# q and k of tiles 8 to 27 turned in 32 by 32 blocks by the vector engine instead of by the tensor engine

## What is computed

```python
for c in range(nc):                       # chunks of 32 tokens
    k_full = concat(mem_k, k[16 tokens before the chunk .. 8 behind it])
    v_full = concat(mem_v, v[the same tokens])
    scores = scale * q_c @ k_full^T
    a = exp(scores - max); a = a / (sum(a) + 1e-9)
    out[chunk] = a @ v_full
x = out, as (3072 tokens, 512)
h = x @ w_in;  solu = h * softmax(h);  ln = (solu - mean) / sqrt(var + 1e-6) * g_ln
x2 = ln @ w_out
h2 = x2 @ w2_in;  g = h2 * clip(h2 + 3, 0, 6) / 6;  result = g @ w2_out
```

## Time and profile before

| | us |
|---|---|
| median of 3 runs | 903.2 |
| lowest and highest | 901.8, 905.31 |
| the profiled execution, its own time | 903.9 |
| its span, from first to last instruction | 901.8 |
| PE busy in the span | 882.5 |
| DVE busy | 677.2 |
| ACT busy | 468.9 |
| POOL busy | 264.4 |

### The profile page before, as it was taken

The page is one execution under the profiler, slowest core; times in us unless marked ns, Lnnn a source line. Parts: engine busy times, 40 slices in busy tenths (PEclk is TensorE's granted clock), DMA queues, the critical chain, the costliest instruction groups (busy, mean ns, idle before and its releaser), DMA issues.

```text
span 901.8 us, 16537 instructions
## 1 busy us (share of the span) xinstructions
PE 882.5 (98%) x6146; PEld 796.7 (88%) x6146; DVE 677.2 (75%) x1100; ACT 468.9 (52%) x1112; POOL 264.4 (29%) x327
## 2 busy tenths in 40 slices
PE   7999999999999999999999999999999999999998
PEld 6788989888988989899888888888799999999998
DVE  5898878888777878757685545555898887979784
ACT  5777565656565654537574555545754333333331
POOL 4473554563341454550122324223610000000000
PEclk9999999999999999999999999999999999999999
DMA  9895265555454464577733333333996435354341
GB/s 211 184 214 127 63 181 164 181 164 179 136 141 131 140 224 133 161 258 275 272 115 133 128 124 129 131 140 115 352 363 238 153 99 159 97 160 142 116 141 47
DMA packets 145017, 149.26 MB, mean 166 GB/s; under 512 B 92725, under 2 KB 104501, under 8 KB 143925
## 3 DMA queue, kind: packets, MB, share of 16 engines
q1 hardware_dynamic: 132205, 103.06, 38.4%
q0 software_dynamic: 7920, 38.94, 12.3%
q10 hardware_dynamic: 4824, 6.34, 2.1%
HBM read 90.77 MB, written 57.54 MB: 164 GB/s over the span
## 4 chain that ended last, share of the span: by engine, by line
PE 85%; DVE 9%; DMA 2%; ACT 2%; issue 1%; SPq 0%; DVEq 0%; ACTq 0%
PE banks L1405 25%; PE banks L1144 24%; PE banks L1096 23%; PE banks L1041 3%; PE banks L1111 3%; DVE prob L1801 2%; PE banks L1049 2%; PE banks L1070 2%; PE banks L993 2%; PE banks L1087 2%; DVE score L1771 1%; DVE small L1779 1%; DMA xs_raw<-x_scratch 1%; DMA gs_raw<-g_scratch 1%; DVE y_t L1762 1%
## 5 line engine op out<-in xcount | busy, mean ns | idle before, releaser
L1405 PE MATMUL banks<-vs,gs 128*128 128x256 f32 x2016 | 242.6, 283 | 1.7 <-DMA vs<-v_split_scratch 1.4
L1405 PEld LDWEIGHTS banks<-vs,gs 128*128 128x128 f32 x2016 | 242.2, 192 | 2.1 <-DVE gs L1762 1.6
L1144 PE MATMUL banks<-xs,ws 128*128 128x512 f32 x1008 | 230.8, 390 | 0.8 <-ACT part L1541 0.8
L1144 PEld LDWEIGHTS banks<-xs,ws 128*128 128x128 f32 x1008 | 188.1, 188 | 42.4 <-issue 2.7
L1719 ACT CAST gs<-gs_raw 128x1792 fp32r<-128x1792 f32 x48 | 81.4, 1696 | 124.3 <-DVE gs_raw L2115 124.3
L1096 PE MATMUL banks<-y_t,w_out 128*128 128x384 f32 x768 | 140.8, 338 | 0.0
L1096 PEld LDWEIGHTS banks<-y_t,w_out 128*128 128x128 f32 x768 | 132.7, 188 | 0.9
L1096 PE MATMUL banks<-w_in,x_t 128*128 128x512 f32 x480 | 114.7, 394 | 0.2 <-DVE solu L1848 0.2
L1488 ACT ACTIVATE prob<-score,small 96x128 f32<-96x128 f32 x256 | 99.3, 392 | 19.1 <-DVE small L1779 17.8
L2115 DVE TENSOR_TENSOR gs_raw<-gs_raw 128x256 f32<-128x256 f32 x192 | 82.1, 428 | 32.3 <-DMA gs_raw<-g_scratch 27.5
L1096 PEld LDWEIGHTS banks<-w_in,x_t 128*128 128x128 f32 x480 | 88.6, 188 | 19.0 <-DVE solu L1848 0.4
(11 more groups left out here) (105 smaller groups left out, 1039.6 us busy)
## 6 DMA issues: line engine op xcount, KB each, us to landing
g_scratch<-part SPq DMA_DIRECT2D x96, 256.0 KB, 2.0
gs_raw<-g_scratch SPq DMA_DIRECT2D x45, 512.0 KB, 4.0
x_scratch<-x_out ACTq DMA_DIRECT2D x32, 192.0 KB, 2.1
v_in<-in_v_dram SPq DMA_DIRECT2D x24, 240.0 KB
out_dram<-o_stage SPq DMA_DIRECT2D x11, 512.0 KB, 5.6
q_in<-in_q_dram SPq DMA_DIRECT2D x28, 192.0 KB, 3.0
v_split_scratch<-v_split POOLq DMA_DIRECT2D x3, 1792.0 KB, 7.7
ws<-w_split_scratch SPq DMA_DIRECT2D x21, 256.0 KB, 5.5
```

Of the source, the lines that this page charges most:

```text
L1144: mm = pe.matmul(ps, ws[:, W_OF[i], a, kc, :], xs[g][X_OF[i]][:, m, kc, :], start=(fresh and x == 0), stop=(x == len(passes) - 1), skip_gr ...
L1405: mm = pe.matmul(m_ps[i][:, s, :], gs[x][:, a, G_OF[i], s * P:(s + 1) * P], vs[p][:, m, V_OF[i], :], start=(p == 0 and s == 0 and y == 0), ...
```

## The change

q and k of tiles 8 to 27 are no longer loaded with tokens on the partitions. A tile of q is loaded by 12 DMAs, one for each of its three chunks of 32 tokens and each of four partition groups (`split_rows`). Group e takes, for every second head, 32 of the 64 features of 32 tokens: 32 partitions (tokens) x 4 head pairs x 32 features, in runs of 128 bytes, 16 KB a DMA. So every 32 by 32 block lies in the partition group in which its transposed values belong. DVE then transposes the blocks in place of their partition group, one instruction for q and one for k (`turn_blocks`), straight into `q_t` and `k_t`. k takes 12 DMAs too, and 24 where a batch begins (tiles 8, 16 and 24), since there the memory rows, the 16 and the 8 rows beside come in DMAs of their own. The DMAs of these 20 tiles are 240 for q and 276 for k; before it was 20 for q and, with 17 joined tiles of which two need a second one, and three whole windows of three, 28 for k.

PE's eight transposes of each of the 20 tiles go, and with them ACT's copies from PSUM. ACT keeps the copy of the 24 old columns (`join_k`). PE's probabilities no longer wait for ACT's copies out of the two banks. The scores of tile n now wait for DVE's blocks of tile n (`blocks_turned`) and for the joined columns.

```diff
+        def by_blocks(n):
+            return TILES <= n < NA - AHEAD
...
+            def split_rows(dst, c, r, src, b, lo, rows, here):
+                for e in range(NQUAD):
+                    sp.dma_start(dst[CHUNK * e + r:CHUNK * e + r + rows, :, c, :],
+                                 src[b, e // 2::2, lo:lo + rows, CHUNK * (e % 2):CHUNK * (e % 2 + 1)]
+                                 .rearrange("h r d -> r h d")).then_inc(here, 16)
...
+                if by_blocks(n):
+                    for c in range(TQ // CHUNK):
+                        split_rows(q_split[t % 2], c, 0, q, b, TQ * t + CHUNK * c, CHUNK, q_in_here[t % 2])
+                    return
...
-                pe.wait_ge(q_in_here[s], 16 * (TILES // 2 * b + t // 2 + 1))
-                turn(turn_ps[0], q_in[:, s], TQ)
-                pe.wait_ge(k_in_here[s], k_in_count(n))
-                if is_joined(n):
-                    turn(turn_ps[1], k_in[0:TQ, s], TQ)
-                else:
-                    turn(turn_ps[1], k_in[:, s], NK)
...
+                elif by_blocks(n):
+                    pe.wait_ge(blocks_turned, 2 * (n - TILES) + 2)
+                    pe.wait_ge(qk_copied, 2 * TILES + joined_before(n + 1))
+                    q_of, k_of = q_t, k_t[n % 2]
...
+            def turn_blocks(n):
+                if not by_blocks(n):
+                    return
+                s = n % 2
+                dve.wait_ge(q_in_here[s], q_in_count(n))
+                dve.wait_ge(scores_done, 2 * n)
+                nc.vector.transpose(q_t[:, :, :].rearrange("p h t -> p (h t)"),
+                                    q_split[s][:, :, :, :].rearrange("p h c d -> p (h c d)")).then_inc(blocks_turned, 1)
+                dve.wait_ge(k_in_here[s], k_in_count(n))
+                cols = slice(NK - TQ if is_joined(n) else 0, NK)
+                nc.vector.transpose(k_t[s][:, :, cols],
+                                    k_split[s][:, :, cols.start // CHUNK:, :].rearrange("p h c d -> p h (c d)")
+                                    ).then_inc(blocks_turned, 1)
...
                 moments_of(3)
+                turn_blocks(TILES)
...
                     if w["own"]:
                         norm_probs(n)
+                        turn_blocks(n + 1)
                     if w["mm1"]:
                         max_hidden(MPG * (i - 1) + u)
```

More of the change, by code:

```diff
@@ L121, in attention_solu_hardswish @@
         k_ahead = [at(f"k_ahead{e}", (198, 200, 202, 188)[e], [P, KD, NK], F32) for e in range(AHEAD)]
+        q_split = [at(f"q_split{s}", 136 + 2 * s, [P, KD, TQ // CHUNK, CHUNK], F32) for s in range(2)]
+        k_split = [at(f"k_split{s}", 140 + 2 * s, [P, KD, NK // CHUNK, CHUNK], F32) for s in range(2)]
         q_back = [at(f"q_back{s}", 136 + 2 * s, [P, KD, TQ], F32) for s in range(2)]
@@ L369, in raw_count, with joined_before, q_loads, q_in_count @@
             return 16 * sum(1 + LOADS[ahead_tile(x)] for x in range(e % 2, e + 1, 2))
+        def by_blocks(n):
+            return TILES <= n < NA - AHEAD
         def is_joined(n):
-            return n >= TILES and n % TILES > 0 and not is_ahead(n)
+            return by_blocks(n) and n % TILES > 0
+        def joined_before(n):
+            return sum(is_joined(x) for x in range(n))
+        def q_loads(n):
+            return 3 * NQUAD if by_blocks(n) else 1
+        def q_in_count(n):
+            return 16 * sum(q_loads(x) for x in range(n % 2, n + 1, 2))
         def k_loads(n):
-            if is_joined(n):
-                return 2 if n % TILES == TILES - 1 else 1
+            if by_blocks(n):
+                return NQUAD * (3 if is_joined(n) else 6)
             return 1 if is_ahead(n) else LOADS[n % TILES]
@@ L473, in load_k @@
                     return
[L474 to L480, removed]
+                if by_blocks(n):
+                    split, here = k_split[t % 2], k_in_here[t % 2]
+                    if t == 0:
+                        split_rows(split, 0, 0, mem_k, b, 0, NMEM, here)
+                        split_rows(split, 0, NMEM, k, b, 0, LEFT, here)
+                        split_rows(split, 0, NMEM + LEFT, k, b, 0, RIGHT, here)
+                    for c in range(TQ // CHUNK):
+                        lo = TQ * t + RIGHT + CHUNK * c
+                        split_rows(split, c + 1, 0, k, b, lo, min(CHUNK, S - lo), here)
                     return
@@ L1051, in turn_half, with turn_probs @@
                 mm.then_inc(prob_turned, 1)
-            def turn_probs(n, behind_qk):
+            def turn_probs(n, banks_read):
                 for half in range(2):
-                    if behind_qk and not is_ahead(n + 1):
-                        pe.wait_ge(qk_copied, 2 * n + 3 + half)
-                    elif not behind_qk and half == 0:
+                    if not banks_read and half == 0:
                         pe.wait_ge(y_lo_done, 2 * MPG * (NG - 1))
@@ L1308, in batch @@
                     if w["own"]:
-                        turn_qk(b if kk else b - 1, (kk - 1) % TILES, i, u)
+                        turns_read(b if kk else b - 1, (kk - 1) % TILES, i, u)
                     if w["mm2"]:
@@ L1662, in batch @@
                         high_x(n - 1, (kk - 2) % TPG, (kk - 2) // TPG % 2)
-                    if not last and not is_ahead(n + 1):
-                        copy_qk(n + 1)
+                    if is_joined(n + 1):
+                        join_k(n + 1)
                     if w["mm1"]:
```

44 lines of the change are left out of this document (21 added, 23 removed).

## The result

The changed kernel takes 954.4 us, the median of four runs (953.3 to 956.3); the kernel before took 903.2 us beside it. The ratio is 1.056, with a 95% interval from 1.053 to 1.059: 51 us slower, where 901.9 us was forecast, and 38 us outside the range. From here on a number such as "1.016 (1.011 to 1.021)" is the ratio to the kernel before on the same chip with its 95% interval, and "+2.3" means 2.3 us later than before.

What follows compares the result with a forecast made beforehand. PE, busy 882.5 of 901.8 us, was taken as the bound. Terms -2.3 + 6.2 - 2.0 - 2.4 + 1.8 gave 1.3 us gained, hence 901.9 us expected as median; range 896 to 916.

Steps and rivals of the forecast that it cites:

- tile 8: Start of tile 8's scores: blocks turned behind the first batch's moments, DVE without slack; a loss of 2.3 us.
- pair 10, 11: Hidden product's end to tile 11's scores, through DVE's moments and a scaling held up by POOL: a loss of 2.0 us.
- pair 14, 15: Scaling as long as tile 10's; maximum 0.7 us later, blocks cost 0.37: a loss of 1.1 us.
- pair 18, 19: Scaling as long as tile 10's; maximum 0.94 us later, blocks cost 0.37: a loss of 1.3 us.
- pairs 22, 23 and 26, 27: Tile pairs free of POOL: a gain of 0.9 us each, 1.8 together.
- The loads: SP's 516 DMAs at 0.36 us an issue, 210 us with v and stores, fit in 257 us: costed at nothing.
- SP becomes the engine that is waited for: Slower rival, SP's queue: at 0.50 us an issue 24 us late, 926 us; at 0.58, 967 us; chance 0.17.
- D: On DVE, how far a tile's two transposes push what stands behind them: 0.94 us, bounds 0.3 to 1.8.
- The clock: Rival: PE idles before tile 8's scores and tile 10's probabilities, clock halves: some 3 us, 905 us; inside the forecast's 0.50.
- covered tiles: Nine tiles where PE's projection hides DVE's turning: each keeps its 0.66 us, 6.2 us gained in all.
- Absorbed delays: Faster rival: pairs lose nothing and each tile but 8 brings 0.66 us; 10 us gained, 893 us; chance 0.16.

Runs made afterwards that it cites:

- two loads, behind scaling: Changed kernel with q and k of tiles 8 to 27 each loaded by one DMA (from w_in, wrong values), turning as changed: 918.3 us, 1.016.
- two loads, narrowed GpSimd: Changed kernel with two loads a tile, turning as changed, GpSimd's mixing and splitting narrowed to 8 columns for all but the first items: 905.2 us, 1.003.
- two loads, idle time: Changed kernel with two loads a tile, both turns moved into DVE's idle stretches: 903.3 us, 1.000.
- shapes run: Kernel before plus 24 unused DMAs a tile in tiles 8 to 27, their rows and runs varied from tile to tile: 958.5 us, single run.
- q alone in idle time: Kernel before with only q of tiles 8 to 27 loaded by blocks and turned by DVE, in DVE's idle time: 902.3 us, 0.998.
- 15 turns: Kernel before with only q of 15 of the 20 tiles loaded by blocks and turned by DVE in idle stretches: 901.6 us, 0.998.

## Why the prediction was wrong, point by point

One table carries most of it: by how much the start of each tile's scores is later than the start of those before it, less the same in the kernel before, in us, from the traces.

| scores of | forecast | two loads, behind scaling | two loads, narrowed GpSimd | two loads, idle time | changed kernel |
|---|---|---|---|---|---|
| tile 8 | +2.3 | +2.3 | +2.3 | +0.1 | +2.3 |
| 9, 12, 13, 16, 17, 20, 21, 24, 25 | -6.2 | +0.8 | -2.9 | -0.4 | +18.8 |
| pair 10, 11 | +2.0 | +1.5 | +1.8 | +0.2 | +5.7 |
| pair 14, 15 | +1.1 | +4.5 | +2.2 | +1.0 | +6.4 |
| pair 18, 19 | +1.3 | +4.2 | -1.7 | +0.9 | +4.4 |
| pairs 22, 23 and 26, 27 | -1.8 | -0.5 | -1.9 | -0.7 | +8.7 |

**The loads: the step that failed.** The prediction wrote: "I take 0.36, since each new DMA stands behind a small one", and costed the loads at nothing with "the cover is 1.3 us there and is gone at 0.38 us an issue". The measured price is 0.475 us in a steady row and 0.533 us on average. The 0.32 us of the rows is the price of an issue behind a pause or behind a DMA of 8 rows, as at line 420; each new load stands behind one of 32 rows, and there the price is 0.43 us and the gap of 0.04. "Small" was taken as the number of runs, which the shapes run shows to count for nothing. The rows of before had a sign of it: q of tile 9, right behind a store, took 0.44 us. The bounds, 0.36 to 0.58, held. (The 2.6 us to landing was the least in its row, whose median is 3.0; the new loads landed in 2.1 us, so that did no harm.) At tile 9, where the working can be followed: the last load of k is issued at 97.3 instead of 85.0. 2.0 us of that is the later start (60.45 for 58.46), 5.8 lie in the first 36 issues (18.8 for 13.0), 1.4 in the eleven others, 3.1 in the 24 of tile 9 (11.7 for 8.6).

**The rival had the mechanism and a price too low.** "SP becomes the engine that is waited for" is what happened, at a chance of 0.17. By its working 0.475 us would be a queue 12 us late. But the 516 issues took 275 us, 0.533 us each on average, since some last up to 2.08 us (30 us in all beyond the steady price), and the 52 other loads and stores between them 0.50 each. From 60.45 us to 361.2 is 301 us where the forecast had 210, and 44 us more than the 257 that the tiles had; the scores of tile 27 start 48.6 us later than before. With 0.533 us the rival's own working gives a queue 42 us late and 944 us; the rest of the 954.4 is no part of it. What makes the long ones long is open. The forecast's rival takes one number for a queue's price; it needed the mean with the stalls in it, not the median. (The 0.68 us that the prediction takes from the Trainium skill, DMA: Bandwidth & Descriptors, "Bandwidth", is there the time of a 4 KB transfer issued by GpSimd, not the price of an issue by SP.)

**D, and tile 8: right.** In the run with two loads q's turn holds back what follows by 0.49 us and k's by 0.46 (durations 0.57 and 0.53 us, medians), D = 0.95 for the forecast 0.94. Here is the wait before the scores of tile 8, 2.9 us forecast:

```profile
84.37 2.02 PE L1069 MATMUL banks<-k_t,q_t 64*96 64x128 f32 x16 [2.75 <-DVE k_t L1818]
```

The term is right to 0.1 us, +2.3. But these scores take 2.02 us where before they took 1.12: the clock has fallen, to 0.50 from 84 to 90 us.

**The clock: right in kind, too small by half or more.** "If it fell to half for 3 us of work each, that would be some 3 us" counted two places. In the run with two loads it fell at five, tiles 8, 11, 15, 19 and 23, each time making the next step 1.2 to 1.6 us longer (tile 9: +0.89, where tile 13 without such a stretch has -0.68), 7 us in all. That is why the covered tiles, forecast at -6.2, came to +0.8. The cover itself held: where the clock stayed up, at tiles 13, 17, 21 and 25, a tile brought 0.68 us, for the 0.66 forecast. The hidden product behind tile 8's wait took 7.05 us there, for 5.74 before.

**The pairs: 10 and 11 right, 14 and 15, 18 and 19 wrong.** +1.5 for the forecast 2.0, with waits of PE of 1.39, 2.00 and 0.40 us at tile 11 where 3 to 4 us were forecast; but +4.5 and +4.2 for 1.1 and 1.3. The prediction took the way from the hidden maximum on as fixed and let the maximum itself come only 0.7 to 0.94 us late. But DVE is held up before it too: GpSimd's mixing waited 2.40 us for its own DMA in the kernel before and started at 149.28, when the first scaling of tile 13 was under way; in the run with two loads the tiles come later and the data is there, so the mixing starts at once, at 156.72, ahead of both scalings. GpSimd there and DVE then:

```profile
156.72 3.19 POOL L871 TENSOR_TENSOR raw_mix<-raw_mix 128x256 f32<-128x256 f32 x4
159.97 0.95 POOL L883 CAST v_split<-raw_mix 128x512 fp32r<-128x512 f32 x1
161.01 1.29 POOL L885 TENSOR_TENSOR v_split<-raw_mix,v_split 128x512 fp32r<-128x512 f32 x1
```

```profile
159.35 1.10 DVE L1831 TENSOR_TENSOR prob<-prob,small 96x512 f32<-96x512 f32 x1
160.38 0.57 DVE L1821 TENSOR_SCALAR small<-small 96x4 f32<-96x4 f32 x1
...
161.19 1.65 DVE L1831 TENSOR_TENSOR prob<-prob,small 96x512 f32<-96x512 f32 x1
162.77 0.56 DVE L1810 STREAM_TRANSPOSE q_t<-q_split 128x384 f32<-128x384 f32 x1
```

In the kernel before the same two scalings took 0.69 and 1.09 us. The hidden maximum starts at 163.72 behind them, though its product ended at 159.4; then ACT's exponential is late, the copy of the probabilities behind it (PE waits 1.73 us at 166.99), and the rest as in the pair 10 and 11. With GpSimd narrowed the pair 18 and 19 goes to -1.7, the forecast's saving without its losses. (The first weights of each kind were left at full width, and GpSimd has them ahead of tiles 11 and 15: these pairs keep +1.8 and +2.2.)

**Absorbed delays: not in this order of work.** In idle time the turning costs nothing (903.3), but the 13.2 us that PE saves come back: as DVE's limit in three pairs, in four stretches of fallen clock, at tiles 11, 15, 19 and 23, and in small waits for probabilities. The PE-only view, "work taken from PE is worth its time there", was the error under the forecast's sign: of what PE saved, no run brought more than some 2 us to the end (0.998 at best, with an interval up to 1.000).

**What stays open.** Tiles 0 to 7, which no kernel here changes, end 2.1 to 3.5 us later than in the kernel before in eight of the traces, the changed kernel's among them, and within 0.9 us of it in the others. In five of the eight the granted clock fell once between 10 and 23 us, in the changed kernel's not. Whether that goes with the program or with the execution was not tried, nor was a second queue for the loads.

## What to carry to other kernels

Before a load is cut into pieces, price an issue by a row of as many as there will be, mean and not median, and multiply by the pieces; here 516 x 0.53 us outgrew the 257 us that the tiles had, and 240 did not. When work moves to an engine that is 80% busy, the instruction's own time tells little; ask at which of its places the engine already stands still, since the same 0.49 us cost 9 us in the wrong place and nothing in the right one. And where two engines already meet at every fourth tile, time taken from one comes back there as a wait, and a wait of under 2 us can cost the clock as well.

## What the hardware showed that was not expected

- Block loads in a row: 0.46 to 0.475 us from start to start for 32 and 16 rows, 0.35 us for 8 rows, and for 32 rows the same for 1, 2 and 4 runs of 128 bytes a row. The first behind a pause or behind a DMA of 8 rows is cheaper, 0.32 us of duration for 0.43.
- A float32 transpose by blocks on VectorE: 0.52 to 0.58 us for 384 columns, 0.66 to 0.71 for 512, 0.46 to 0.49 us from the start of one of 384 to what follows, and not stretched by GpSimd. The Trainium skill, VectorE: DVE Perf Modes, "The three transpose paths", led to an estimate of some 0.6 us in the prediction, and the trace agrees.
- The smallest instructions are not safe beside GpSimd: 1.76 us for 96x4 values instead of 0.17.
- The granted clock fell to about half (1.2 GHz; 0.50 to 0.62 in the stretches read) at PE's waits of 2.75 us, and behind pairs of waits such as 0.24 and 1.67. Behind others it went either way: with q alone in idle time it held behind waits of 1.71 and 1.83 us and fell behind another of 1.71; with 15 turns it held behind 0.24 and 1.34 and fell behind 0.24 and 1.21.
